# A second batch's attention placed between the first layer's units, in two PSUM banks

## The chip, the cores and the metric

The kernel runs on one core of one Trainium2 chip. The metric is the device time of one execution in microseconds; lower is better.

## The reference

Attention over two batches with 8 heads, 576 tokens and 64 values a head, then two dense layers over all 1152 tokens. Cut to what matters:

```python
q_d, k_d, v_d = means of 4 neighbouring tokens                # 144 tokens
out_up    = repeat(softmax(q_d k_d^T / 8) v_d, 4)
out_local = softmax(q k^T / 8 where |i - j| < 4) v
x = (out_up + out_local), heads side by side                  # [1152, 512]

h = x @ w_in1; P = a0 + a1 h + a2 h^2 + a3 h^3
x = (P / (1 + |b0| |h| + |b1| h^2 + 1e-6)) @ w_out1           # 512 -> 2048 -> 512
h = x @ w_in2; out = (h * tanh(softplus(h))) @ w_out2
```

## The kernel before

**Attention.** Eight steps, each of them one pair of heads of one batch (steps 0 to 3 are batch 0, steps 4 to 7 batch 1). All of it is float32. One step on TensorE (PE): `turn_q` and `turn_k` transpose q and k (L399); `score_local` makes the banded scores in 36 small products (L422); `score_down` those of the pooled tokens (L432); `turn_p` transposes the local weights (L443) and `turn_d` the pooled ones (L454); `out_down` (L463) and `out_local` (L475, 36 small products) make the outputs. ScalarE (ACT) copies each of the transposed things out of PSUM (`put`, L565) and takes the exponentials. VectorE (DVE) pools q and k (L722), adds the mask and takes off the maximum (`shift_local` L741 to L744, `shift_down` L757 and L760), sums (L766 to L768), adds the two outputs (`join`, L793) and makes the float16 rest of x (`x_rest`, L799). GpSimd (POOL) pools v and normalises (L925, L930).

**The plan.** `STAGES` names for each stage its engine and its tick within a step, a step starts every 10 ticks, and each engine's queue is this list in order of ticks. A stage that writes PSUM opens one or more jobs; the jobs take the banks 0 to 6 in turn, and a job waits until the one that held its bank before has been emptied. Bank 7 is for `keep_busy`: filler matmuls of the identity that feed nothing (L392). They stand at the start and in the first and the last step.

**Weights.** A unit is a 128 x 1024 piece of `w_in` (even numbers) or `w_out` (odd). SyncE (SP) loads it, ACT makes its float16 head (L622), DVE makes the rest of an even unit (L839), POOL that of an odd one in two halves (L938, L940). 13 units are made during the attention, the others during the first layer.

**Layers.** They begin when all eight steps are through (`x_rest_put` at 8). The tokens are cut in blocks (layer one: 256, 256, 256, 192, 192), the work in 80 tiles. For tile m, `hidden(m)` makes h in one of two banks (24 products, L498); ACT, DVE and POOL make g out of it in a chain (`first_reads`, `fraction`, `estimate`, `quotient`, `head`, `rest`); `output_first(m)` multiplies by `w_out` (L519), `output_second` in layer two (L539). PE's queue is `hidden(0..3)`, and then `output(m)`, `hidden(m + 4)` in turn. `hidden(m)` waits for `h_done` of tile m - 2, which DVE gives with the last `fraction` part (L828). At the end of a block the sums leave as the next layer's x (L676, L870).

## Time and profile before

| | us |
|---|---|
| three timed runs | 530.66, 531.88, 538.64 (median 531.88) |
| the profiled execution | 529.39, its span 527.6 |
| first matmul of the layers starts | 129.11 |
| first output of layer one starts | 147.10 |
| busy in the span: PE, DVE, ACT, POOL | 507.1, 391.0, 305.6, 194.7 |

The span goes from the first to the last instruction; the execution's time has 1.8 us more around it. PE is TensorE's matmul row, PEld its weight loads, which overlap with it. The granted clock is a share of 2.4 GHz: 1.00 is 2.4 GHz and 0.50 is 1.2 GHz. The starts of PE's rows are measured, their ends modelled, so neighbouring rows overlap a little; what a stage takes is read from start to start.

### The profile page before, as it was taken

How to read it: one execution, taken by the hardware profiler on the slowest of the kernel's cores; microseconds unless marked ns; L12 is line 12 of the kernel's file. 1: busy time of each engine (PE TensorE's matmuls, PEld its weight loads, DVE VectorE, ACT ScalarE, POOL GpSimd, SP SyncE). 2: the span in 40 equal slices, each digit the busy share in tenths (PEclk: the TensorE clock that was granted, in tenths of full speed). 3: DMA queues.
4: the chain of work that ended last, by engine and by line, in shares of the span. 5: the costliest groups of instructions: out<-in, count | busy, mean ns of one | idle time of the engine just before them, and what ended most of it. 6: DMA issues, size and time to landing. Idle time of an engine off the chain costs nothing.

```text
span 527.6 us, 11364 instructions
## 1 busy us (share of the span) xinstructions
PE 507.1 (96%) x4566; PEld 378.8 (72%) x4566; DVE 391.0 (74%) x670; ACT 305.6 (58%) x553; POOL 194.7 (37%) x204
## 2 busy tenths in 40 slices
PE   7999999999799989989999999999999999999995
PEld 5788888886588878878989989744444555557762
DVE  1687674552688887887888887887787888787873
ACT  2465463331878668786787878454545455545542
POOL 6486663320167242551542554312121222221221
PEclk8795755555899999999999999999999999999999
DMA  7999893111111211202112100000000020000101
GB/s 166 217 216 203 185 170 96 28 42 73 48 40 41 81 44 38 81 4 79 41 41 81 42 1 1 1 1 1 1 0 1 0 81 1 1 1 0 61 2 40
DMA packets 45572, 29.72 MB, mean 56 GB/s; under 512 B 30928, under 2 KB 39120, under 8 KB 45520
## 3 DMA queue, kind: packets, MB, share of 16 engines
q1 hardware_dynamic: 44344, 28.71, 22.1%
q8 instruction: 36, 0.59, 0.5%
q10 hardware_dynamic: 1176, 0.30, 0.3%
q14 instruction: 16, 0.13, 0.1%
HBM read 26.64 MB, written 2.36 MB: 55 GB/s over the span
## 4 chain that ended last, share of the span: by engine, by line
PE 50%; issue 29%; POOL 10%; DVE 5%; ACT 3%; DMA 1%; ACTq 0%; POOLq 0%; DVEq 0%
PE bank L498 15%; PE bank L519 14%; POOL g_l L953 9%; PE bank L422 5%; PE bank L475 5%; PE bank L443 3%; PE bank L399 2%; PE bank L392 2%; PE bank L432 1%; PE bank L463 1%; DMA late<-in_k 1%; PE bank L454 1%; PE bank L539 1%; ACT work L644 1%; DVE x_l L870 1%
## 5 line engine op out<-in xcount | busy, mean ns | idle before, releaser
L953 POOL TENSOR_TENSOR g_l<-work,g_h 128x512 f16<-128x512 f32 (+1 forms) x80 | 85.9, 1074 | 271.1 <-ACT g_h L668 253.4
L498 PE MATMUL bank<-x_h,w 128*128 128x256 f16 (+1 forms) x640 | 104.0, 266 | 4.6 <-DVE work L828 3.4
L519 PE MATMUL bank<-g_h,w 128*128 128x256 f16 (+1 forms) x640 | 101.2, 262 | 0.3 <-POOL g_l L953 0.3
L498 PE MATMUL bank<-x_h,late 128*128 128x512 f16 (+2 forms) x384 | 96.8, 326 | 0.0
L539 PE MATMUL bank<-late,g_h 128*128 128x512 f16 x288 | 92.1, 379 | 1.5 <-POOL g_l L953 1.5
L658 ACT ACTIVATE bank<-work,coef 128x512 f32<-128x512 f32 (+1 forms) x80 | 52.1, 652 | 69.1 <-DVE work L824 66.1
L498 PE MATMUL bank<-x_l,w 128*128 128x256 f16 (+1 forms) x320 | 85.3, 267 | 0.0
L519 PE MATMUL bank<-g_l,w 128*128 128x256 f16 (+1 forms) x320 | 83.8, 262 | 0.0
L498 PEld LDWEIGHTS bank<-x_h,w 128*128 128x128 f16 x640 | 61.9, 99 | 11.1 <-DVE work L828 4.0
L519 PEld LDWEIGHTS bank<-g_h,w 128*128 128x128 f16 x640 | 60.9, 98 | 6.6 <-issue 1.3
L498 PE MATMUL bank<-x_l,late 128*128 128x512 f16 (+2 forms) x192 | 62.6, 326 | 0.0
L814 DVE SCALAR_TENSOR_TENSOR work<-work,coef 128x512 f32<-128x512 f32 (+1 forms) x40 | 30.3, 758 | 38.7 <-ACT work L644 38.7
L565 ACT ACTIVATE late<-bank 128x288 f32<-128x288 f32 (+2 forms) x80 | 30.6, 426 | 45.4 <-PE bank L454 19.1
L498 PEld LDWEIGHTS bank<-x_h,late 128*128 128x128 f16 x384 | 37.6, 98 | 26.0
L539 PE MATMUL bank<-late,g_l 128*128 128x512 f16 x144 | 54.6, 379 | 0.0
L539 PEld LDWEIGHTS bank<-late,g_h 128*128 128x128 f16 x288 | 28.2, 98 | 34.8 <-POOL g_l L953 2.5
L848 DVE SCALAR_TENSOR_TENSOR work<-work,bank 128x512 f32<-128x512 f32 (+1 forms) x80 | 50.1, 626 | 0.0
L852 DVE SCALAR_TENSOR_TENSOR work<-work,bank 128x512 f32<-128x512 f32 (+1 forms) x80 | 49.9, 623 | 0.0
L641 ACT ACTIVATE work<-bank 128x512 f32<-128x512 f32 (+1 forms) x40 | 22.2, 555 | 45.2 <-PE bank L498 44.9
L668 ACT ACTIVATE g_h<-work 128x512 f16<-128x512 f32 (+1 forms) x80 | 47.0, 588 | 2.3 <-DVE work L861 2.2
L824 DVE SCALAR_TENSOR_TENSOR work<-work 128x512 f32<-128x512 f32 (+1 forms) x40 | 47.9, 1197 | 0.0
L817 DVE TENSOR_SCALAR work<-work 128x512 f32<-128x512 f32 (+1 forms) x40 | 16.0, 400 | 34.5 <-ACT work L649 34.5
(92 smaller groups left out, 860.0 us busy)
## 6 DMA issues: line engine op xcount, KB each, us to landing
late<-in_v SPq DMA_DIRECT2D x16, 288.0 KB
raw<-in_moe_w_out SPq DMA_DIRECT2D x8, 512.0 KB, 3.8
raw<-in_moe_w_in SPq DMA_DIRECT2D x7, 512.0 KB, 3.6
work<-in_moe_w_in SPq DMA_DIRECT2D x5, 512.0 KB, 6.4
late<-in_moe_w_out SPq DMA_DIRECT2D x5, 512.0 KB, 3.9
out<-w SPq DMA_DIRECT2D x9, 256.0 KB, 2.8
late<-in_q SPq DMA_DIRECT2D x15, 144.0 KB
late<-in_k SPq DMA_DIRECT2D x15, 144.0 KB
```

The source lines that it names most:

```text
L422: last = pe.matmul(ps[32 * g:32 * g + 32, KW * u:KW * (u + 1)], q_t[s % 2][h0:h0 + 64, QT * t:QT * (t + 1)], k_t[s % 2][h0:h0 + 64, QT * t ...
L498: last = pe.matmul(ps, w_in(l, wp)[:, kk, at], x[:, kk, t0:t0 + n], start=(kk == 0 and wp == 0 and x is x_h), stop=(kk == KD - 1 and wp == 1))
L519: last = pe.matmul(ps, w_out(0, wp)[:, f, 128 * d:128 * (d + 1)], g[q % 4][:, i * n:(i + 1) * n], start=False, stop=(f == FT - 1 and d % 2 ...
L539: last = pe.matmul(y2_bank[row % 4][:, :], g[q % 4][:, i * n + 128 * t:i * n + 128 * (t + 1)], w_out(1, wp)[:, f, :], start=(f == 0 and wp ...
L565: act.activation(dst, src, ACT.Copy, scale=scale).then_inc(act_emptied, 1)
L658: act.activation(r, den[q % 3][:, 0:w], ACT.Ln, bias=(one_eps, two)[layer]).then_inc(ln_done, 1)
L668: act.activation(g_h[q % 4][:, 0:w], num[q % 4][:, 0:w], ACT.Copy).then_inc(g_head, 1)
L814: dve.scalar_tensor_tensor(out=d, in0=d, scalar=b1_abs, in1=ab[q % 2][:, 0:w], op0=ALU.mult, op1=ALU.add).then_inc(den_done, 1)
L824: dve.scalar_tensor_tensor(out=d, in0=d, scalar=2.0, in1=d, op0=ALU.add, op1=ALU.mult).then_inc(den_done, 1)
L848: dve.scalar_tensor_tensor(out=d, in0=d, scalar=(Q_ONE, 2.0)[layer], in1=r, op0=ALU.add, op1=ALU.mult).then_inc(nt_done, 1)
L852: dve.scalar_tensor_tensor(out=d, in0=d, scalar=(2.0, 2.0 * K2)[layer], in1=r, op0=ALU.subtract, op1=ALU.mult).then_inc(nr_done, 1)
L953: pool.tensor_tensor(g_l[q % 4][:, 0:w], num[q % 4][:, 0:w], g_h[q % 4][:, 0:w], ALU.subtract).then_inc(g_rest, 1)
```

## The change

Four parts, in the code's order.

1. The plan has one list for everything: attention stages, loads, heads and rests of weight units. Each engine goes through its part of it with `Schedule.until(tick)`. The layers begin at tick 60.5 (`LAYERS`); the four units of the ramp are 0.94 ticks apart, and each slot of `output(m)`, `hidden(m + 4)` takes 2.5 ticks. Stages of later ticks stand between those units on every engine: the tails of steps 4 and 5 and nearly all of 6 and 7.
2. Jobs before tick 56.25 take banks 0 to 6 in turn, later ones banks 6 and 7 only, since the layers need 0 to 5.
3. `hidden(0)` waits for four steps of x, not eight, and tile 16, the first with tokens of batch 1, for all eight.
4. Filler matmuls follow `score_local` (3), `out_local` (3) and its first half (3) in every step that stands before the layers, and every stage of step 0 (4). In all there are 92 fillers, 84 before. `turn_p` is three jobs of 4, 4 and 1 transposes, k is loaded and turned ahead of q, and units 7 and 9 are made during the layers: five odd units in slots 1 to 5.

The diff, cut:

```diff
-    EARLY_OUT = 5
-    SLOTS = (6, 4)
+    EARLY = [0, 1, 2, 3, 4, 5, 6, 8, 10, 12, 14]
+    LATER = [7, 9, 11, 13, 15] + [FT + i for i in range(FT)]
...
+    LAYERS, PREFILL, SLOT = 60.5, 3.75, 2.5
+    TWO_BANKS = LAYERS - 4.25
...
-              ("pe", "score_down", 9),
...
+              ("pe", "score_down", 6),
...
+    def pe_tick(p):
+        return LAYERS + PREFILL + SLOT * p
+    def other_tick(m, part):
+        return max(LAYERS + PREFILL * (m + 2) / 4 + part, pe_tick(m - 3 + part))
...
-            bank = n_jobs % 7
+            if tick < TWO_BANKS:
+                bank, n_early = n_early % 7, n_early + 1
+            else:
+                bank, n_late = 6 + n_late % 2, n_late + 1
...
+            def until(self, tick):
+                while self.done < len(self.todo) and self.todo[self.done][0] < tick:
+                    _, stage, i = self.todo[self.done]
+                    stage(i)
+                    self.done += 1
...
+                    if j == 0 and PERIOD * s + 21 < TWO_BANKS:
+                        keep_busy(3)
+            def with_filler(stage, times):
+                at = next(t for _, name, t in STAGES if name == stage.__name__)
+                def run(s):
+                    stage(s)
+                    if PERIOD * s + at < TWO_BANKS:
+                        keep_busy(4 if s == 0 else times)
+                return run
...
                 if q == 0:
-                    pe.wait_ge(x_rest_put, STEPS)
+                    for bank in range(6):
+                        wait_emptied(pe, holder_at_switch[bank])
+                    pe.wait_ge(x_rest_put, PAIRS)
+                elif l == 0 and f0 == 0 and t0 + n > S:
+                    pe.wait_ge(x_rest_put, STEPS)
...
-            for _, i, s in plan:
-                if STAGES[i][0] == "pe":
-                    stages[STAGES[i][1]](s)
-                    if s == 0 or s == STEPS - 1:
-                        keep_busy(4)
+            schedule = Schedule("pe", stages)
             for m in range(LAG):
+                schedule.until(LAYERS + PREFILL * m / 4)
                 hidden(m)
             for m in range(NT):
+                schedule.until(pe_tick(m))
                 (output_first, output_second)[tiles[m][0]](m)
                 if m + LAG < NT:
+                    schedule.until(pe_tick(m + 0.5))
                     hidden(m + LAG)
```

In the changed kernel the same operations have other lines. On PE: turns L416, score_local L440, score_down L450, turn_p L459, turn_d L478, out_down L487, out_local L499, fillers L409, hidden L541, output_first L562. On DVE: pooling L771, shift_local L790 to L793, shift_down L806 and L809, join L842, x_rest L848; the fraction's parts L869, L876, L883.

PE's queue where step 2 goes over to step 3, before: the turns, the local output in two halves, turn_p.

```order
L399 MATMUL bank2<-ident,late 128x72 x4
L399 MATMUL bank3<-ident,late 128x72 x4
L475 MATMUL bank4<-late 64x32 x18
L475 MATMUL bank5<-late 64x32 x18
L443 MATMUL bank6<-ident,late 38x128 x3
L443 MATMUL bank0<-ident,late 38x128 x3
```

The same place now:

```order
L416 MATMUL bank2<-ident,late 128x72 x4
L416 MATMUL bank3<-ident,late 128x72 x4
L499 MATMUL bank4<-late 64x32 x18
L409 MATMUL bank7<-ident 128x256 x3
L499 MATMUL bank5<-late 64x32 x18
L409 MATMUL bank7<-ident 128x256 x3
L459 MATMUL bank6<-ident,late 38x128 x4
```

Fillers stand after each half of the local output.

PE's queue from turn_d(5) to the turn of k for the last step, before:

```order
L454 MATMUL bank5<-ident,late 72x72 x4
L454 MATMUL bank6<-ident,late 72x72 x4
L432 MATMUL bank0<-late 72x144
L432 MATMUL bank1<-late 72x144
...
L399 MATMUL bank2<-ident,late 128x72 x4
L399 MATMUL bank3<-ident,late 128x72 x4
```

Now, between hidden(4) and output(1):

```order
L478 MATMUL bank7<-ident,late 72x72 x4
L478 MATMUL bank6<-ident,late 72x72 x4
L450 MATMUL bank7<-late 72x144
L450 MATMUL bank6<-late 72x144
...
L416 MATMUL bank7<-ident,late 128x72 x4
L416 MATMUL bank6<-ident,late 128x72 x4
L562 MATMUL bank4<-g_h1,w1 128x256
```

Three stages that had six banks now have two, so each stage waits for the emptying of the one ahead of it.

DVE's queue at the start of the layers, before: the fraction of tile 0 behind all of the attention.

```order
L799 SCALAR_TENSOR_TENSOR x_l<-late,x_h 128x576
L889 TENSOR_SCALAR coef<-coef 128x1 x4
...
L814 SCALAR_TENSOR_TENSOR work<-work,coef 128x512
L821 TENSOR_TENSOR work<-work,bank 128x512
L828 SCALAR_TENSOR_TENSOR work<-work,coef,bank 128x512
L814 SCALAR_TENSOR_TENSOR work<-work,coef 128x512
```

Now:

```order
L869 SCALAR_TENSOR_TENSOR work<-work,coef 128x512
L842 TENSOR_TENSOR late<-bank7,late 128x288
L842 TENSOR_TENSOR late<-bank6,late 128x288
L771 TENSOR_REDUCE late<-late 128x144
L876 TENSOR_TENSOR work<-work,bank0 128x512
L883 SCALAR_TENSOR_TENSOR work<-work,coef,bank0 128x512
L869 SCALAR_TENSOR_TENSOR work<-work,coef 128x512
L897 SCALAR_TENSOR_TENSOR work<-work,bank2 128x512
L848 SCALAR_TENSOR_TENSOR x_l<-late,x_h 128x576
```

The join of step 4, the pooling of k for step 6 and x_rest(4) stand between the parts of tiles 0 and 1, ahead of the operations that give h_done.

## Rows read from the trace of the kernel before

**Rows 1.** The page: span, engine PE, and the granted clock in 40 slices

```profile
span 527.6 us, 11364 instructions
...
PE 507.1 (96%) x4566; PEld 378.8 (72%) x4566; DVE 391.0 (74%) x670; ACT 305.6 (58%) x553; POOL 194.7 (37%) x204
...
PEclk8795755555899999999999999999999999999999
```

**Rows 2.** Table of stretches: us, busy us of PE, PEld, DVE, ACT, POOL, clock, DMA share, GB/s

```profile
19.50:39.98 20.48, 19.43 (x392) 17.04 (x393) 17.36 (x36) 14.16 (x33) 17.26 (x18) 1.00 0.98 208
39.98:60.46 20.48, 20.37 (x253) 17.21 (x250) 14.10 (x29) 11.36 (x23) 15.40 (x17) 0.50 0.91 185
60.46:67.30 6.84, 6.84 (x160) 6.18 (x159) 5.04 (x12) 3.90 (x12) 1.89 (x3) 1.00 0.87 205
67.30:129.10 61.80, 60.60 (x700) 49.78 (x697) 32.18 (x71) 23.03 (x49) 20.55 (x21) 0.50 0.36 77
129.10:147.10 18.00, 14.58 (x98) 10.73 (x99) 10.43 (x21) 12.12 (x19) 3.50 (x4) 0.82 0.17 59
147.10:181.30 34.20, 34.20 (x315) 30.64 (x315) 28.13 (x40) 26.26 (x44) 17.54 (x17) 1.00 0.21 63
147.10:527.60 380.50, 369.65 (x2841) 265.36 (x2840) 306.12 (x487) 236.30 (x416) 127.93 (x121) 1.00 0.09 28
```

**Rows 3.** PE's timeline at full clock, step 2's group and what stands before it

```profile
20.79 1.16 PE L443 MATMUL bank<-ident,late 128*38 128x128 f32 x9 [0.79 <-POOL late L925]
...
28.70 2.29 PE L475 MATMUL bank<-late 38*64 38x32 f32 x72
30.92 0.61 PE L392 MATMUL bank<-ident 128*128 128x256 f16 x4
31.37 1.15 PE L443 MATMUL bank<-ident,late 128*38 128x128 f32 x9
32.44 2.39 PE L422 MATMUL bank<-late 64*32 64x38 f32 x72
34.76 0.78 PE L454 MATMUL bank<-ident,late 72*72 72x72 f32 x8
35.47 0.71 PE L432 MATMUL bank<-late 64*72 64x144 f32 x8
...
36.76 0.71 PE L463 MATMUL bank<-late 72*64 72x144 f32 x8
```

**Rows 4.** The same timeline at half clock: turn_p of two steps, one row of fillers

```profile
41.24 2.10 PE L443 MATMUL bank<-ident,late 128*38 128x128 f32 x9
...
56.99 2.11 PE L443 MATMUL bank<-ident,late 128*38 128x128 f32 x9
...
92.70 1.06 PE L392 MATMUL bank<-ident 128*128 128x256 f16 x4
93.69 1.23 PE L463 MATMUL bank<-late 72*64 72x144 f32 x8
```

**Rows 5.** Table of stretches: one attention step at full clock

```profile
24.69:34.94 10.25, 10.25 (x207) 9.02 (x208) 8.63 (x19) 6.56 (x14) 9.26 (x11) 1.00 0.93 192
```

**Rows 6.** Waits of PE: us in total, times, longest

```profile
PE bank L513 <- DVE x_l L870: 4.8, 4, 1.5
PE bank L498 <- DVE work L828: 3.4, 2, 2.4
```

**Rows 7.** Groups of instructions: DVE and ACT in the whole span, POOL in 147.1 to 181.3

```profile
L565 ACT ACTIVATE late<-bank 128x288 f32<-128x288 f32 (+2 forms) x80 | 30.6, 426 | 45.4 <-PE bank L454 19.1 <-PE bank L443 19.0 <-PE bank L399 5.4
...
L757 DVE TENSOR_REDUCE small<-bank 72x2 f32<-72x288 f32 x16 | 6.5, 446 | 2.7 <-PE bank L432 2.6
...
L839 DVE SCALAR_TENSOR_TENSOR w<-raw,w 128x1024 f16<-128x1024 f32 x3 | 3.6, 1191 | 0.0
...
L940 POOL TENSOR_TENSOR w<-raw,w 128x512 f16<-128x512 f32 x3 | 4.0, 1333 | 0.2
...
L938 POOL TENSOR_SCALAR raw<-raw 128x512 f32<-128x512 f32 x3 | 2.7, 909 | 0.0
```

More of the change, by code:

```diff
@@ L103, in attention_moe_moe @@
-    plan = sorted((PERIOD * s + t, i, s) for s in range(STEPS) for i, (_, _, t) in enumerate(STAGES))
-    JOBS = {"turn_q": 2, "turn_k": 2, "score_local": 1, "score_down": 2, "turn_p": 3, "turn_d": 2,
+    LAYERS, PREFILL, SLOT = 60.5, 3.75, 2.5
+    TWO_BANKS = LAYERS - 4.25
+    STAGES = [("sp", "load_qk", -16),
+              ("pe", "turn_k", -4),
+              ("act", "put_k", -2),
+              ("pe", "turn_q", 0),
+              ("act", "put_q", 0),
+              ("dve", "pool_q", 2),
+              ("dve", "pool_k", 3),
+              ("sp", "load_v", 4),
+              ("pe", "score_local", 4),
+              ("pe", "score_down", 6),
+              ("dve", "shift_local", 6),
+              ("act", "exp_local", 7),
+              ("dve", "shift_down", 8),
+              ("act", "exp_down", 10),
+              ("sp", "load_windows", 10),
+              ("pool", "norm_local", 10),
+              ("dve", "sum_local", 10),
+              ("dve", "sum_down", 12),
+              ("pe", "turn_p", 12),
+              ("pool", "norm_down", 14),
+              ("act", "put_p", 14),
+              ("pe", "turn_p_end", 14),
+              ("act", "put_p_end", 16),
+              ("act", "put_d", 16),
+              ("pe", "turn_d", 16),
+              ("pool", "pool_v", 17),
+              ("pe", "out_down", 19),
+              ("act", "put_down", 20),
+              ("pe", "out_local", 21),
+              ("dve", "join", 23),
+              ("act", "x_head", 23),
+              ("dve", "x_rest", 24)]
@@ L108, in attention_moe_moe @@
+    for i, u in enumerate(LATER):
+        slot = 1 + i if u < FT else 24 + 1.5 * (u - FT)
+        events += [(pe_tick(slot - 3) - 3, "sp", "load_unit", u), (pe_tick(slot - 2.25), "act", "head_unit", u),
+                   (pe_tick(slot - 2), REST_ENGINE[u % 2], "rest_unit", u)]
+    plan = sorted(events, key=lambda event: event[0])
+    JOBS = {"turn_q": 2, "turn_k": 2, "score_local": 1, "score_down": 2, "turn_p": 2, "turn_p_end": 1, "turn_d": 2,
             "out_down": 1, "out_local": 2}
-    DVE_EMPTIES = ("score_local", "score_down", "out_local")
+    EMPTIES = {"put_q": "turn_q", "put_k": "turn_k", "shift_local": "score_local", "shift_down": "score_down",
+               "put_p": "turn_p", "put_p_end": "turn_p_end", "put_d": "turn_d", "put_down": "out_down", "join": "out_local"}
@@ L119, in attention_moe_moe @@
             job = (name, s, j)
-            bank_of[job], place[job], emptied[job] = bank, n_jobs, (by, counts[by])
+            bank_of[job], place[job] = bank, n_early + n_late
             before[job] = holder.get(bank)
             holder[bank] = job
+        for j in range(JOBS[EMPTIES[name]] if name in EMPTIES else 0):
+            freed[eng] += 1
+            emptied[(EMPTIES[name], s, j)] = (eng, freed[eng])
+    holder_at_switch = {bank: job for job, bank in bank_of.items() if bank < 6}
@@ L596, in put_p, with put_p_end @@
                     act.wait_ge(job_filled, place[("out_local", s - 1, 1)])
[L597 to L599 removed]
+                put_p_job(s, "turn_p", 0, 0, 4)
+                put_p_job(s, "turn_p", 1, 4, 4)
+            def put_p_end(s):
+                put_p_job(s, "turn_p_end", 0, 8, U - 8)
             def put_d(s):
@@ L893, in _ @@
             dve.memset(ln_k, math.log(K2)).then_inc(coefs, 1)
+            schedule.until(LAYERS)
             dve.wait_ge(coefs, 8)
@@ L898, in _ @@
                 for part in range(3):
+                    schedule.until(other_tick(m, 0.6 + 0.33 * part))
                     if m < NT:
```

203 lines of the change are left out of this document (84 added, 119 removed).

## The prediction

> **What bounds the kernel now.** I read the page's first lines and its forty slices, then a table of stretches, then TensorE's and VectorE's timelines, and last the waits. [rows 1]: PE is busy for 96% of a span of 527.6 us, so nothing counts that doesn't shorten PE's own time. The clock row says how: it stands at 5 in slice 4 and in slices 6 to 10, and at 9 from slice 12 on. [rows 2] gives the same by stage. In 39.98 to 60.46 and in 67.30 to 129.10 PE is busy almost throughout (20.37 of 20.48 us, 60.60 of 61.80) at a granted clock of 0.50, the lower level (1.2 GHz); from 147.10 on it is 1.00. So up to 129.10 the attention is bound by PE at half its clock. After 147.10 the layers are bound by PE at full clock: 369.65 of 380.50 us busy.
>
> **What an attention step costs PE.** One step (two heads) at full clock, by starts in [rows 3]: nine transposes of the local weights 31.37 to 32.44 = 1.07 us; the local scores (L422) 2.32; turn_d (L454) 0.71; score_down (L432) and one turn (L399) 35.47 to 36.76 = 1.29, and out_down (L463) and the other turn, which are as long, 1.29; the local output (L475) 28.70 to 30.92 = 2.22. Sum 8.9 us. At half clock [rows 4] a step goes from 41.24 to 56.99 = 15.75 us. Eight steps are 71 us at full clock; the old kernel takes 129.1.
>
> **The change, part by part.** Three things happen: filler matmuls of ident into bank 7 stand in every step before the layers, not only in the first and last; the plan is cut at tick 60.5, where the layers begin; and what is left of the attention is put between their units, in banks 6 and 7.
>
> (1) *The stretch up to the first layer matmul.* In the old kernel turn_p (L443) of steps 0, 1 and 2 starts at 20.79, 31.37 and 41.24 [rows 3, 4]: 10.6 and 9.9 us a step at full clock, though PE needs only 8.9. VectorE explains it: in one such step (24.69 to 34.94) it is busy 8.63 of 10.25 us, and the DMA engines 0.93 of it [rows 5], 0.98 over 19.50 to 39.98 [rows 2]. In the new order turn_p(4) is followed by the rest of that group up to the second half of turn_q(6), then hidden(0). The step's price: PE 8.9 us and 9 fillers (3 after score_local, 3 and 3 around the second half of out_local; four in 31.37 - 30.92 = 0.45 us, so 0.11 each) = 9.9 us. VectorE 8.63 us with one weight rest of 1.19 (L839 [rows 7]), and two of them in steps 3 to 5, since all eight even units still go to it before the layers: about 9.8. DMA as dense as it was, since the unit loads are two a step as before; it gave 10.2 us a step. Three resources within 5% of each other queue behind each other, so I take 11.0. Bounds 10.25 (the old pace) and 12.4 (PE at half clock for a third of the time, 9.9 + 1/3 of the 7 us that half clock adds). First layer matmul: 20.8 + 4 x 11.0 + 7.1 (1.07 + 2.32 + 0.71 + 0.64 + 3 x 0.65 for out_down and two turns, 0.4 of filler; each piece from [rows 3]) = **71.9 us**, bounds 69 and 78, in place of 129.1. Gain 57.2 us.
>
> That the clock stays up there is an assumption, and the largest one. For it: from 19.50 to 39.98 it was 1.00 [rows 2] through four rows of four fillers, the last at 30.92, and it lasted 9 us beyond that one. It fell at 39.98, right after 36 small output products with a pause in them, and at 67.30, again at the end of such a row. Exactly this row is now broken by fillers. Against it: four fillers in 1 us at 92.70 [rows 4], and seven more such rows up to 127, did not lift it from 0.50.
>
> A rule speaks against the step as well. With no filler anywhere near, the clock went to 1.00 at 60.46, after 2 us of 128x128 transposes and 1.4 us of score products, and stood there for 6.84 us [rows 2]. The Trainium skill, "TensorE: Matmul & The Clock Gate", Part 4: PE-mode transpose, says the opposite of transposes: the full clock "doesn't engage" for them, as they don't count as a busy PE. By that rule the 33 transposes of a step would work against the fillers and the half clock would stay until the layers, which is rival A; the row shows that it can't hold strictly.
>
> (2) *The ramp of the layers.* Before, 129.10 to 147.10 = 18.0 us for four units, at a mean clock of 0.82 [rows 2]; four units at full clock are 4 x 2.62 = 10.5 us. The rest is waiting for h_done (3.4 us [rows 6]), the entry, and half clock. Now out_local(4) (2.22), turn_p(5) (1.07) and score_local(6) (2.32) stand in those gaps: 5.6 us of work. 10.5 + 5.6 + 0.5 = 16.6 is the floor; I keep **18.0 us**, as the third and fourth unit still wait for VectorE, which now has join(4), pool_k(6) and x_rest(4) between its fractions. Bounds 16.6 and 22. No gain in length, but 5.6 us of attention is done in it.
>
> (3) *What the layers now carry.* At PE tick 60.5 there remain 2 turns, 2 score_local, 2 score_down, 3 turn_p, 3 turn_d, 3 out_down, 4 out_local: 1.3 + 4.64 + 1.28 + 3.21 + 2.13 + 1.92 + 8.88 = 23.4 us at full clock. Less the 5.6 in the ramp: **+17.8 us**. It is spread over slots 0 to 10, about 4 slots a step. Does another engine become the bound? In 147.10 to 181.30 a tile takes 5.24 us of PE; DVE, ACT and POOL are busy 28.13, 26.26 and 17.54 of 34.20 [rows 2], that is 4.3, 4.0 and 2.7 us a tile. Four slots with a step are 21.0 + 8.9 = 29.9 us of PE, against DVE 17.2 + 7.5 = 24.7 (83%) and ACT 16.1 + 6 = 22 (74%). POOL 10.8 + 5 and, in slots 1 to 5, one odd weight unit each (2 x (0.9 + 1.33) us by L938 and L940, [rows 7]) where it had one in two: 1.2 for g's rest, 4.5 and 1.3, some 7.0 of 7.5 us. So PE stays the bound, but POOL is close to full for five slots, and some of the waits below may come from there.
>
> (4) *New waits.* The two banks cost PE a round trip wherever two stages stand together. That is so once at its worst: turn_d(5), score_down(6), turn_k(7) without a unit between them. score_down needs turn_d's banks back (two copies, 0.43 us each) and turn_k needs shift_down, four VectorE operations of 0.45 us [rows 7] behind whatever tile operation stands ahead: 1 + 3 us. turn_d(6) with score_down(7): 1 us. Behind a waiting PE stand output(1) and hidden(5), and behind these all engines. Elsewhere a unit of 2.62 us lies between, and in-order DVE, ACT and POOL will still be late at times: of the 37 late jobs I give 3 us in all. **+8 us**, bounds 2 and 20 (nearest rows: no wait over 0.8 us for a bank or a normalised tile in the old attention, and 0.98 and 2.4 us for h_done in the ramp).
>
> (5) *The rest.* 147.10 to 527.60 = 380.5 us stays, with its boundary waits (4.8 us for y, [rows 6]); the order of loads (k first, coefficients earlier) and the split 4+4+1 of turn_p move nothing that PE waits for longer than now. At nothing.
>
> Sum by the profiled execution: 71.9 + 18.0 + 17.8 + 8 + 380.5 = 496.2 us of span, and 529.39 - 527.6 = 1.8 around it: 498.0. The three timed runs lay at 530.66, 531.88 and 538.64, 1.3 us and more above the profiled one, so I forecast **499 us** as their like (-6%).
>
> **Rivals.** *A: the clock stays at half until the layers.* The fillers of 92 to 127 speak for it. A step then costs 15.75 + 9 x 0.24 = 17.9 us (a filler at half clock: 93.69 - 92.70 = 0.99 for four), PE being the bound again: 4.7 steps x (17.9 - 11.0) = +32: 531 us, no change. Partly so, one or two of five steps: 505 to 518.
> *B: the attention's jobs hold PE in the layers.* This one ends slower. Every one of the 37 jobs between PE's units needs its bank back from ACT or DVE, and its input by way of a chain DVE, ACT, DVE, POOL, each in order behind tile work; POOL's 4.5 us weight unit may stand ahead of a normalisation for which turn_p or turn_d waits. It decides from 1.4 us a job (50 us: 498 - 8 + 50 = 540, slower by 2%); at 2 us it is 564. Against it: the page of before shows 0.3 to 0.8 us for such waits on PE, and a tick is 2 to 3 us long in the layers.
> *C: better than forecast.* VectorE and the loads keep 10.25 us a step, the boundary wait after the first block is filled with steps 6 and 7, and only two of the bank waits show: 484 to 488.
>
> **How the numbers follow.** The forecast with its bounds, 488 to 505: 0.57. Partly half clock, or waits towards 20 us, 505 to 518: 0.19. A, 518 to 534: 0.10. B above 540: 0.05. C below 488: 0.09. The range 486 to 518 leaves out some 2 in 10. A measurement of this kernel tells 2%, 10.6 us, from no change; below 521 counts as faster: 0.86, same 0.09, slower 0.05.
>
> **What would show it.** The clock 1.00 in most slices from 20 us on; the first L541 at 69 to 78 us; the first L562 some 18 us after; PE busy above 96% between them and slot 11, with one wait of 3 us for shift_down (L809) at turn_k(7). A clock of 0.50 in slices 3 to 6 means A. POOL or DVE named as releaser of L459, L478, L450 or L416 in the layers, with over 1 us each, means B.

## The result, and the profile after

The changed kernel took **518.35 us** (median of four executions, 511.29 to 523.62; two more took 515.84 and 523.88) beside 531.27 us for the kernel before on the same chip: a ratio of **0.967, interval 0.960 to 0.974**. Forecast were 499 us and 486 to 518. The direction is right. The point is 19 us too low, and this median lies 0.35 us above the upper end of the range; the ratio, 0.967 of 531.27, stands for 513.7 us, which is inside it. The profiled execution took 523.14 us, at the long end of the changed kernel's times. A second profile of the same kernel, taken among the experiments, is of an execution of 514.24 us; the two are read side by side. The ratios and their intervals leave out executions more than 1.5% above the fastest of their kernel, while the medians and ranges given here are over all executions; since part of that scatter is the kernel's own clock, as will be seen, both are given.

The page of the changed kernel: span, engines, and the granted clock in 40 slices of 13.0 us.

```profile
span 521.3 us, 11406 instructions
...
PE 492.1 (94%) x4574; PEld 363.2 (70%) x4574; DVE 392.9 (75%) x670; ACT 305.6 (59%) x553; POOL 191.3 (37%) x204
...
PEclk9887655999999899999999999989999999999999
```

Beside [rows 1], PE is busy 15.0 us less and idle 8.7 us more. The clock is no longer at 5 for six slices, but it isn't at 9 from 20 us on either: it sinks from 8 in slices 2 and 3 through 7 and 6 to 5 in slices 6 and 7. Later there are two more 8s, in slices 14 and 27, which the old kernel doesn't have.

The table of stretches of the changed kernel, in the columns of [rows 2]. The cuts are 60 us, the first layer matmul (L541), the first output matmul of layer one (L562), the first output matmul of layer two (L582) and the end.

```profile
20.00:60.00 40.00, 38.91 (x620) 32.05 (x618) 29.52 (x66) 21.34 (x45) 21.97 (x25) 0.80 0.90 197
60.00:88.20 28.20, 28.20 (x318) 23.70 (x318) 15.40 (x32) 11.12 (x25) 6.64 (x8) 0.50 0.61 131
88.20:109.30 21.10, 19.42 (x255) 15.91 (x254) 14.89 (x24) 15.60 (x28) 10.12 (x11) 0.88 0.20 61
109.30:334.40 225.10, 213.42 (x2268) 187.10 (x2268) 176.37 (x289) 155.96 (x284) 90.53 (x89) 0.99 0.16 44
334.40:521.30 186.90, 178.67 (x960) 93.94 (x960) 145.98 (x235) 92.04 (x159) 49.90 (x47) 0.99 0.05 16
```

The same table of the second profile of this kernel:

```profile
20.00:60.00 40.00, 38.33 (x721) 33.00 (x723) 35.51 (x73) 25.98 (x56) 27.93 (x28) 0.96 0.90 200
60.00:82.10 22.10, 20.06 (x233) 16.57 (x230) 13.45 (x30) 8.72 (x21) 5.02 (x7) 0.59 0.85 167
82.10:101.80 19.70, 18.02 (x253) 15.15 (x251) 14.82 (x24) 15.50 (x27) 10.55 (x11) 0.94 0.23 59
101.80:325.40 223.60, 211.90 (x2267) 186.40 (x2266) 176.44 (x289) 156.09 (x284) 90.64 (x89) 1.00 0.15 45
325.40:512.40 187.00, 178.71 (x960) 94.02 (x960) 145.92 (x235) 92.16 (x160) 49.95 (x47) 0.99 0.05 16
```

And the kernel before, cut at its first output matmul of layer two (345.20), since the prediction had only the sum of the two:

```profile
147.10:345.20 198.10, 192.59 (x1881) 171.80 (x1881) 163.84 (x256) 147.39 (x260) 86.75 (x82) 1.00 0.14 41
345.20:527.60 182.40, 177.06 (x961) 93.57 (x959) 142.29 (x232) 88.91 (x157) 41.18 (x39) 1.00 0.04 14
```

So the sum of the prediction stands against the first profile like this:

| us | before | forecast | after | after, second profile |
|---|---|---|---|---|
| to the first layer matmul | 129.1 | 71.9 | 88.2 | 82.1 |
| ramp | 18.0 | 18.0 | 21.1 | 19.7 |
| layer one from there | 198.1 | 198.1 + 17.8 + 8 = 223.9 | 225.1 | 223.6 |
| layer two | 182.4 | 182.4 | 186.9 | 187.0 |
| span | 527.6 | 496.2 | 521.3 | 512.4 |

The misses are 16.3 + 3.1 + 1.2 + 4.5 = 25.1 us. Two thirds lie before the first layer matmul, in the stretch whose clock was assumed. There the fillers do break the row of output products, as meant; a piece of PE's timeline around 56 us, where the clock falls to half, shows it:

```profile
53.89 1.24 PE L499 MATMUL bank<-late 38*64 38x32 f32 x36
55.06 0.50 PE L409 MATMUL bank<-ident 128*128 128x256 f16 x3
55.49 2.03 PE L499 MATMUL bank<-late 38*64 38x32 f32 x36
57.45 0.82 PE L409 MATMUL bank<-ident 128*128 128x256 f16 x3
58.06 2.13 PE L459 MATMUL bank<-ident,late 128*38 128x128 f32 x9
```

The first 36 output products take 1.24 us, the next 36 take 2.03, and the nine transposes 2.13 instead of 1.15: the clock falls in the middle of the row, between two groups of fillers. It goes up and down: full from 21.5 to 32, 35.5 to 42 and 49 to 56 us, half between and from 56 to 93.5. The second profile has other steps (full 20 to 43.5 and 47 to 64, half until 84.5), with the same instructions in the same order.

### The profile page after: what moved, and what is told of

Its sections match the earlier page's. It is cut to its first block, busy times and chain, and to the rows that moved or that the text cites. A ratio compares the mean times of both kernels' runs of the same rounds, so it can differ in the third digit from the quotient of the medians.

```text
span 521.3 us, 11406 instructions
## 1 busy us (share of the span) xinstructions
PE 492.1 (94%) x4574; PEld 363.2 (70%) x4574; DVE 392.9 (75%) x670; ACT 305.6 (59%) x553; POOL 191.3 (37%) x204
## 4 chain that ended last, share of the span: by engine, by line
PE 50%; issue 24%; POOL 11%; DVE 7%; ACT 5%; DMA 1%; ACTq 0%; POOLq 0%; DVEq 0%
PE bank L541 17%; PE bank L562 14%; POOL g_l L1001 8%; PE bank L499 4%; PE bank L440 4%; PE bank L582 2%; PE bank L459 2%; PE bank L409 2%; PE bank L416 2%; DMA late<-in_q 1%; ACT late L673 1%; DVE x_l L919 1%; PE bank L450 1%; DVE work L869 1%; PE bank L487 1%
## 5 line engine op out<-in xcount | busy, mean ns | idle before, releaser
L562 PE MATMUL bank<-g_h,w 128*128 128x256 f16 (+1 forms) x640 | 102.6, 264 | 2.6 <-POOL g_l L1001 2.6
L541 PE MATMUL bank<-x_h,w 128*128 128x256 f16 (+1 forms) x640 | 103.5, 266 | 1.7 <-DVE work L883 1.7
L582 PE MATMUL bank<-late,g_h 128*128 128x512 f16 x288 | 92.8, 382 | 4.9 <-DVE x_l L919 2.9
L541 PE MATMUL bank<-x_h,late 128*128 128x512 f16 (+2 forms) x384 | 97.2, 327 | 0.0
L541 PE MATMUL bank<-x_l,w 128*128 128x256 f16 (+1 forms) x320 | 85.0, 266 | 0.0
L562 PE MATMUL bank<-g_l,w 128*128 128x256 f16 (+1 forms) x320 | 84.4, 264 | 0.0
L562 PEld LDWEIGHTS bank<-g_h,w 128*128 128x128 f16 x640 | 61.3, 98 | 11.8 <-POOL g_l L1001 4.4
L541 PEld LDWEIGHTS bank<-x_h,w 128*128 128x128 f16 x640 | 61.8, 99 | 7.3 <-DVE work L883 2.2
L541 PE MATMUL bank<-x_l,late 128*128 128x512 f16 (+2 forms) x192 | 62.8, 327 | 0.0
L869 DVE SCALAR_TENSOR_TENSOR work<-work,coef 128x512 f32<-128x512 f32 (+1 forms) x40 | 34.8, 870 | 32.2 <-ACT work L691 32.0
L541 PEld LDWEIGHTS bank<-x_h,late 128*128 128x128 f16 x384 | 37.7, 98 | 26.6 <-issue 0.8
L582 PEld LDWEIGHTS bank<-late,g_h 128*128 128x128 f16 x288 | 28.3, 98 | 39.1 <-POOL g_l L1001 3.6
L607 ACT ACTIVATE late<-bank 128x288 f32<-128x288 f32 (+3 forms) x80 | 31.3, 425 | 40.8 <-PE bank L478 29.0
L582 PE MATMUL bank<-late,g_l 128*128 128x512 f16 x144 | 55.1, 382 | 0.0
L879 DVE SCALAR_TENSOR_TENSOR work<-work 128x512 f32<-128x512 f32 (+1 forms) x40 | 44.7, 1117 | 0.0
L872 DVE TENSOR_SCALAR work<-work 128x512 f32<-128x512 f32 (+1 forms) x40 | 17.9, 448 | 30.8 <-ACT work L696 30.8
```

Source lines behind the costliest of these rows:

```text
L541: last = pe.matmul(ps, w_in(l, wp)[:, kk, at], x[:, kk, t0:t0 + n], start=(kk == 0 and wp == 0 and x is x_h), stop=(kk == KD - 1 and wp == 1))
L562: last = pe.matmul(ps, w_out(0, wp)[:, f, 128 * d:128 * (d + 1)], g[q % 4][:, i * n:(i + 1) * n], start=False, stop=(f == FT - 1 and d % 2 ...
L582: last = pe.matmul(y2_bank[row % 4][:, :], g[q % 4][:, i * n + 128 * t:i * n + 128 * (t + 1)], w_out(1, wp)[:, f, :], start=(f == 0 and wp ...
L607: act.activation(dst, src, ACT.Copy, scale=scale).then_inc(act_emptied, 1)
L869: dve.scalar_tensor_tensor(out=d, in0=d, scalar=b1_abs, in1=ab[q % 2][:, 0:w], op0=ALU.mult, op1=ALU.add).then_inc(den_done, 1)
L879: dve.scalar_tensor_tensor(out=d, in0=d, scalar=2.0, in1=d, op0=ALU.add, op1=ALU.mult).then_inc(den_done, 1)
```

## The experiments

All ratios are against the kernel before in the same set of runs, whose medians were 530.15, 530.47 and 532.5 us. In the first of these sets (no_fill, fill8, units_early, old_fill) the old kernel itself scattered: six of its 17 executions took 517.95 to 524.98 us, at a mean granted clock of 0.922 to 0.941 over the span, and the others 528.04 to 540.19 us at 0.886 to 0.916. The ratios of that set lean on the shorter ones (fill8's is 0.973, where the medians give 0.967), so they are not compared to the per cent with ratios of the other two sets. The milestones of a run (first layer matmul, ramp, layer one, layer two) are those of the table above, from its profile.

**Do the fillers hold the clock, or does nothing?** The first run leaves out the added fillers (those of step 0 stay, as in the old kernel); the second puts eight where three stood.

```
no_fill                                          fill8
- keep_busy(3)                                   - keep_busy(3)
+ keep_busy(3 if s == 0 else 0)                  + keep_busy(8)
- score_local=with_filler(score_local, 3)        - score_local=with_filler(score_local, 3)
+ score_local=with_filler(score_local, 0)        + score_local=with_filler(score_local, 8)
- out_local=with_filler(out_local, 3)            - out_local=with_filler(out_local, 3)
+ out_local=with_filler(out_local, 0)            + out_local=with_filler(out_local, 8)
```

> The changed kernel without its fillers from step 1 on (step 0 keeps its fours). Theory 1, the clock: the profiled execution lost 16 us to my forecast ahead of the layers because PE ran at 0.50 from 56 to 93 us in spite of the fillers. If the fillers buy any clock at all, taking them away puts the half clock over nearly all of 31 to 93 us: first layer matmul at 92 to 100 us, time 520 to 530. Rival 1, the fillers buy nothing and only cost PE time (9 a step, 0.24 us each at half clock): first layer matmul 4 to 8 us earlier than 88 us, time 505 to 515.

Measured: 519.4 us, ratio 0.985 (0.976 to 0.995); first layer matmul at 85.3. Without fillers the first layer matmul comes 2.9 us earlier than in the first profile with them and 3.2 us later than in the second. It lies between the two forecasts (92 to 100 us, and 4 to 8 us before 88). The stretches of this kernel:

```profile
24.00:41.00 17.00, 17.00 (x347) 14.85 (x344) 14.15 (x31) 10.99 (x25) 13.64 (x15) 0.99 0.81 196
41.00:85.30 44.30, 44.30 (x531) 37.88 (x530) 28.96 (x66) 20.45 (x44) 13.49 (x15) 0.50 0.79 163
```

and its PE timeline at the end of its longest stretch at full clock:

```profile
32.15 0.61 PE L409 MATMUL bank<-ident 128*128 128x256 f16 x4
32.60 1.15 PE L459 MATMUL bank<-ident,late 128*38 128x128 f32 x9
33.67 2.38 PE L440 MATMUL bank<-late 64*32 64x38 f32 x72
...
39.27 2.96 PE L499 MATMUL bank<-late 38*64 38x32 f32 x72
```

Four groups of step 0 stand between 25.9 and 32.8; from there on there is no filler, and for 8 us more only transposes and small products run, at a mean of 0.98; only the last part of the 72 output products at 39.27 slows down (2.96 us where full clock gives 2.29, [rows 3]). So this small work can keep the clock for a while by itself. From 20 us to its first layer matmul this execution was at half clock for 48 us, more than in six of the seven profiles with nine fillers a step (14 to 44 us, table further down); by the line through those, 48 us would put the first layer matmul at 90 us. So the 33 fillers that are left out here seem to have bought some clock and to have cost about as much PE time, 4 to 8 us at 0.11 to 0.24 us each.

> The changed kernel with 8 fillers in place of 3 at each of the three places of a step. Theory 1: a denser PE keeps 1.00 for most of the stretch; PE then needs 8.9 + 24 x 0.11 = 11.6 us a step and the first layer matmul stands at 74 to 80 us, time 505 to 512 with little scatter. Rival 1, the filler does not hold the clock: a step at half clock is 15.75 + 24 x 0.24 = 21.5 us, first layer matmul beyond 98 us, time 525 to 540.

Measured: 512.64 us, ratio 0.973 (0.964 to 0.982); 508.45 profiled. Its stretches:

```profile
20.00:74.70 54.70, 54.65 (x1000) 47.34 (x999) 43.90 (x96) 31.78 (x70) 29.49 (x31) 1.00 0.93 205
74.70:93.30 18.60, 16.92 (x253) 14.58 (x253) 15.12 (x26) 15.67 (x28) 11.11 (x11) 1.00 0.32 82
93.30:319.70 226.40, 214.94 (x2268) 187.98 (x2268) 176.30 (x289) 155.94 (x284) 90.70 (x89) 0.98 0.15 43
319.70:506.60 186.90, 178.68 (x960) 93.98 (x960) 145.93 (x235) 92.06 (x159) 49.88 (x47) 0.99 0.04 16
```

This is the assumption of step (1) made true: the clock is 1.00 from 20.5 us through the ramp. The steps take 11.7 us (turn_p at 31.85, 43.55, 55.22, 66.92) with 24 fillers, where I had put 11.0 with nine; the first layer matmul comes at 74.7. The ramp, 21.1 us at 0.88, is 18.6 at 1.00. Layers one and two are as in the changed kernel, so what they lose has nothing to do with the clock of the attention. But three of its six times are above 515 us (515.27, 517.47, 523.19). The mean granted clock over the span is on record for each execution: 0.969, 0.962 and 0.959 for these three, 0.978 to 0.985 for the other three. So it is the clock that varies, and even eight fillers hold it in some executions only.

**More groups of fillers instead of thicker ones.** A group of three or four behind every PE stage, 30 a step.

```
- keep_busy(4 if s == 0 else times)
+ keep_busy(4 if s == 0 else 3)
```

> The changed kernel with 3 fillers behind every stage of every step before the layers (30 a step, not 9). Theory 1b: the fillers hold the clock if none of the small products goes on for long without them; then the clock is 1.00 from 20 us on, a step costs 8.9 + 3.3 = 12.2 us and the first layer matmul stands at 76 to 82 us in every execution: times 507 to 514, a scatter of some 5 us. If the clock still falls, a step at half clock is 23 us and times go up to 540.

Measured: 515.2 us, ratio 0.967 (0.962 to 0.973); first layer matmul 81.4. The theory fails: the clock still fell twice (at 44.5 and at 58 us, for 3.5 us each), and one execution took 569.28 us at a mean granted clock of 0.836. A step at full clock is about 12.6 us long (turn_p at 32.51 and 45.07), where 12.2 were expected. 24 fillers in thick groups did better in the profile (74.7); against nine (77.1 to 93.2 in seven profiles) thirty show no clear gain or loss.

**The other half of the change: fillers without interleaving.** The old kernel, whose attention is finished before the layers, with fillers in steps 1 to 6: three, and eight. (As the code cut shows, the group within out_local stands in all eight steps.)

```
 for j in range(2):                 # out_local of the old kernel
+    if j == 0:
+        keep_busy(3)               # 8 in the other run
...
+ elif STAGES[i][1] in ("score_local", "out_local"):
+     keep_busy(3)                  # 8 in the other run
```

> The old kernel with only the fillers of the change (3 after score_local, 3 within and 3 after out_local in steps 1 to 6). Theory 1, with mixed clock as in the changed kernel (1.00 for some 60% of 20 to 60 us and then half): attention ends 5 to 15 us earlier, time 517 to 527. If the fillers do nothing for the clock: 6 x 9 x 0.24 = 13 us longer, 540 to 545. From this and the changed kernel follows what the interleaving alone is worth.

Measured: 524.35 us, ratio 0.966 (0.955 to 0.977), but single executions from 505.73 to 539.26; the medians over all executions give 0.989. Its shortest execution is below the shortest of the interleaved kernel with the same nine fillers (507.17 of twelve), and its median above both of that kernel's (518.35, 514.27). The profiled one (537.65) had the first layer matmul at 138.0, later than without fillers, as a part of its stretches shows:

```profile
21.00:79.00 58.00, 58.00 (x642) 47.55 (x642) 28.45 (x59) 23.49 (x49) 31.90 (x35) 0.50 0.74 164
79.00:86.00 7.00, 7.00 (x144) 5.94 (x140) 4.96 (x12) 4.15 (x11) 0.71 (x2) 0.98 0.40 113
86.00:138.00 52.00, 49.62 (x760) 41.07 (x760) 31.49 (x71) 22.03 (x49) 20.72 (x21) 0.76 0.30 69
```

58 us at 0.50 with the same nine fillers a step that I had counted on. An execution of 505.73 us of the same program is 32 us shorter; it left no trace, but its mean granted clock was 0.976, where the profiled one had 0.911. Nine fillers don't hold the clock reliably.

> The old kernel, attention whole ahead of the layers, with 8 fillers at the three places of steps 1 to 6. It tells what the interleaving is worth once the clock holds: 20.8 + 7 x 11.6 + 10 = 112 us to the first layer matmul, 18.0 of ramp and 380.5: 510 to 515. The changed kernel with 8 fillers had a median of 512.6. So I expect the two to be within 1%: the interleaving gains some 37 us ahead of the layers and gives back 29 in layer one and 4.5 in layer two.

Measured: 516.46 us, ratio 0.971 (0.966 to 0.977); 513.35 profiled.

```profile
20.00:114.50 94.50, 92.74 (x1640) 79.23 (x1638) 65.23 (x141) 47.91 (x107) 54.24 (x56) 0.96 0.70 150
114.50:131.00 16.50, 13.09 (x98) 10.02 (x98) 10.41 (x21) 12.11 (x19) 3.47 (x4) 0.90 0.20 65
131.00:329.20 198.20, 192.66 (x1882) 171.80 (x1882) 163.92 (x256) 147.60 (x260) 86.75 (x82) 1.00 0.14 41
329.20:511.50 182.30, 177.01 (x961) 93.58 (x959) 142.27 (x232) 88.91 (x157) 41.23 (x39) 1.00 0.04 14
```

Against fill8 this gives what interleaving is worth where fillers hold the clock in both: the first layer matmul comes 39.8 us earlier, and it is paid back with 2.1 us in the ramp, 28.2 in layer one and 4.6 in layer two. 4.9 us of span are left, and 3.8 us between the medians (512.64 and 516.46, from two sets of runs), 0.7%; the two ratios, 0.973 and 0.971, don't tell them apart. These 4.9 us are not idle time that was filled: PE is idle for 26.8 us of fill8's span and for 20.5 of this one, 6.3 more. It is busy for 479.8 us in place of 491.0, and 92 fillers fewer (152, not 244; 0.11 us each) are 10.1 of these 11.2 us. The work moved runs on PE either way; with the clock held, interleaving saves only fillers.

**Where layer one and two lose.** Here I had several candidates: layer-two units prepared too late or in the wrong place (three runs), the five odd units of layer one that crowd POOL and ACT in slots 1 to 5, and turn_k(7) directly behind score_down(6).

```
- slot = 1 + i if u < FT else 24 + 1.5 * (u - FT)
+ slot = 1 + i if u < FT else 16 + 1.4 * (u - FT)          # units_early
+ slot = 1 + 1.5 * i if u < FT else 24 + 1.5 * (u - FT)    # odd_spread
+ slot = 1 + i if u < FT else 14 + 2 * (u - FT)            # units_two
+ slot = 1 + i if u < FT else 15 + 2 * (u - FT)            # units_odd
```

> The changed kernel, but layer two's 16 weight units are made in slots 16 to 37 of the plan, not 24 to 46.5. In the profiled execution PE stood still for 2.5 us in 290 to 300 and 3.4 us in 329 to 345, with a unit's head on ACT in the chain both times; the old kernel had finished its units by then. Theory 2: the late units cost layer one's end and layer two's start 4 to 6 us; time 506 to 512. Rival 2: the same stalls come with the units wherever they stand (the old kernel had 10.9 us of them over the layers), time unchanged within 2 us.

Measured: 527.78 us, ratio 0.999 (0.990 to 1.008). The windows of its layers:

```profile
99.20:334.60 235.40, 217.38 (x2267) 189.99 (x2267) 182.73 (x293) 159.40 (x286) 99.41 (x97) 0.97 0.15 44
334.60:517.00 182.40, 177.04 (x961) 93.59 (x959) 142.34 (x232) 88.88 (x157) 41.21 (x39) 1.00 0.04 14
```

Layer two is back at the 182.4 of the old kernel, to the tenth: the 4.5 us that it loses in the change are those of units prepared in slots 24 to 46, some of which run into it. By the two tables 2.9 of them are PE idle (8.2 us, 5.3 in the old kernel) and 1.6 PE busy for longer: behind the wait of 2.95 us at 338.77 the granted clock is 0.76 over 340 to 345. But layer one is 10.3 us longer than in the change, a larger price than the one saved: 6.3 us of it idle, with waits for g_l of up to 3.7 us, and 4.0 busy at a mean clock of 0.97. Both forecasts fail, since the stalls moved with the units and grew.

> The changed kernel with units 7, 9, 11, 13 and 15 at slots 1, 2.5, 4, 5.5 and 7 in place of 1 to 5. In the first profile output(2) started at 124.84, after a chain put_d on ACT, weight head, two weight halves and pool_v on POOL (115.6 to 123.6), then g's rest; PE stood for 2.3 us in 109.3 to 125. Theory 3 (POOL's queue): the wait goes for the most part, from first output of layer one to first of layer two 221 to 223 us in place of 225.1. Rival 3 (the wait comes from PE's own stall at the two banks, which started the chain late): 224 to 226 us.

Measured: 519.99 us, ratio 0.971 (0.967 to 0.974); layer one 227.3 us, layer two 186.9. Spreading the odd units saves nothing in layer one (2.2 us more than in the change). The theory that they crowd it falls. The trace of the changed kernel had said so: in 115.6 to 124.8, where POOL works through the two halves of such a unit and a pooling, PE waited for POOL only 0.22 us.

The waiting rows of PE's timeline in layer one of the changed kernel are few (the group in brackets is the idle time before the row):

```profile
115.88 0.71 PE L450 MATMUL bank<-late 64*72 64x144 f32 x8 [0.67 <-ACT late L607]
...
117.99 0.74 PE L416 MATMUL bank<-ident,late 72*128 72x72 f32 x8 [1.40 <-DVE late L809]
...
124.84 0.28 PE L562 MATMUL bank<-g_h,w 128*128 128x256 f16 x1 [0.22 <-POOL g_l L1001]
...
148.13 0.71 PE L450 MATMUL bank<-late 64*72 64x144 f32 x8 [0.67 <-ACT late L607]
...
171.30 1.11 PE L556 MATMUL bank<-zeros 32*128 32x512 f16 x2 [2.58 <-DVE x_l L919]
```

The 1.40 us is the wait that step (4) named, turn_k(7) for the subtractions of shift_down, at half its forecast price. The next run puts turn_k(7) 1.5 ticks and put_k(7) one tick later.

```
+ shift = {("turn_k", 7): 1.5, ("put_k", 7): 1}
- events = [(PERIOD * s + t, eng, name, s) ...
+ events = [(PERIOD * s + t + shift.get((name, s), 0), eng, name, s) ...
```

> The changed kernel with turn_k of the last step 1.5 ticks later, behind output(1) and no longer directly behind score_down(6), and put_k a tick later. Theory 4: of my 5 us for the two-bank round trips only 2.7 us were seen (0.67, 1.40, 0.67); moving the turn takes away the 1.40 and at most what hangs on it: the stretch from first output of layer one to first of layer two 222 to 224 us. Rival 4: POOL's chain is the later of the two, nothing changes (225 us).

Measured: 521.44 us, ratio 0.966 (0.962 to 0.971); layer one 226.9 us. The wait itself is gone, and others have come, further down the same timeline:

```profile
117.82 0.67 PE L417 MATMUL bank<-ident,late 72*128 72x72 f32 x8
...
122.44 0.71 PE L488 MATMUL bank<-late 72*64 72x144 f32 x8 [1.32 <-issue]
...
123.51 0.28 PE L563 MATMUL bank<-g_h,w 128*128 128x256 f16 x1 [0.36 <-POOL g_l L1002]
```

1.40 us removed; 1.32 us are new, and the wait for g_l has grown from 0.22 to 0.36. The wait was a place where PE waited for the slower engines, not the cause of their being late.

**Preparation of layer-two units behind the copies of a block end.** The chain of work at the start of layer two in the changed kernel (start, us, what) shows why PE waits there:

```profile
333.51 0.44 ACT x_h L723
...
334.25 1.07 ACT late L673
...
335.49 1.00 issue
...
337.78 0.95 DVE x_l L919 x2
...
338.77 2.59 PE bank L582 x6
```

L723 is the copy of the block's new x on ACT; directly behind it in ACT's queue stands L673, the rounded head of a weight unit, 1.07 us. The harm is done on VectorE, in the time that this chain calls issue. Its queue has the rest of that unit (L855) ahead of the last work on the tile and of the block's x_l (L919):

```profile
335.35 1.23 DVE L855 SCALAR_TENSOR_TENSOR late<-raw,late 128x1024 f16<-128x1024 f32 x1 [2.59 <-ACT late L673]
```

DVE stands for 2.59 us until the head is there, works 1.23 us on the rest, and only then goes on to what PE needs. PE's L582 waits 2.95 us in the end. If this is a mechanism, then units in slots 14, 16, ... 44, which put such a head behind the copies at four of five block ends, should lose in layer one, and units in slots 15, 17, ... 45, with none there, should not.

> The changed kernel with layer two's units at every second slot, 14 to 44, not every 1.5 slots from 24. With units at 16 + 1.4 k layer two took 182.4 us as in the old kernel, but layer one 235.4 in place of 225.1. Theory 5, density: ACT needs 3.3 us a tile of 192 tokens and 1.05 us a unit against 3.97 us of PE, so a unit every 1.5 tiles makes ACT and DVE the bound there and one in two tiles does not: layer one 220 to 224 us, layer two 182 to 185, together 4 to 8 us less than 412. Rival 5, place: units in the slots that follow the attention hurt whatever their spacing, and layer one is 228 us or more.

Measured: 532.2 us, ratio 0.989 (0.983 to 0.994); layer one 240.4, layer two 185.7. PE's waits in this kernel (total, times, longest):

```profile
PE bank L556 <- DVE x_l L919: 12.0, 4, 3.5
PE bank L562 <- POOL g_l L1001: 5.0, 6, 1.5
```

> The changed kernel with layer two's units at every second slot as before, but at 15, 17, ... 45, so that no weight head comes directly behind the ACT copies that end a block (it did at four of five block ends of layer one with 14, 16, ... 44). Theory 6, collision: a unit's head (1.05 us on ACT) behind the end of a block delays the next tile's h_done, the y rest and g's rest, and that, not the density, made layer one 240.4 us; now layer one 218 to 222 us, layer two 182 to 184, so the time from first layer matmul to the end is 422 to 427 us against 430 to 433 in the changed kernel. Theory 5 (density alone): the same 240 us, as the density is the same.

Measured: 515.59 us, ratio 0.966 (0.960 to 0.972); layer one 229.4, layer two 183.2.

```profile
PE bank L556 <- DVE x_l L919: 6.5, 4, 2.6
...
PE bank L562 <- POOL g_l L1001: 2.0, 2, 1.0
```

One slot's shift of the same work takes 11.0 us off layer one. The two waits fall by 8.5 us (12.0 to 6.5 and 5.0 to 2.0); PE's whole idle time in it falls by 6.5 (19.9 to 13.4), and its busy time by 4.5 (220.5 to 216.0), at mean clocks of 0.96 and 0.98. Density alone would have changed nothing, so the collision is real and costs about 2 us a block end (8.5 over four) and what follows of lower clock. As in the changed kernel it is VectorE's queue that passes it on. At the second block end units_two has the unit's rest between the tile's work and x_l, and in units_odd no unit stands there:

```profile
215.89 1.23 DVE L855 SCALAR_TENSOR_TENSOR late<-late 128x1024 f16<-128x1024 f32 x1 [1.77 <-ACT late L673]
...
218.36 1.28 DVE L919 SCALAR_TENSOR_TENSOR x_l<-bank,x_h 128x512 f16<-128x512 f32 x2
```

The runs don't separate the head on ACT from the rest on DVE, since a shift moves both. But I had expected 218 to 222 us of layer one, and 229.4 came; so theory 6 names a cause and overrates it. Layers one and two together are 412.6 us here and 412.0 and 410.6 in the two profiles of the changed kernel: the change as it was has a head behind the copies at one block end only, so there was little to save. The late places cost 4.5 us in layer two, the earlier ones 4.3 in layer one.

**The best of both, and the changed kernel once more.** units_odd with the eight fillers of fill8:

> The same with 8 fillers in place of 3 at the three places of a step. With the first layer matmul at 75 to 85 us, as with 8 fillers before, and 422 to 427 us behind it: 500 to 512 us. If theory 6 fails it is 508 to 523 as with 8 fillers alone.

Measured: 509.38 us (504.81 to 515.57), ratio **0.956 (0.951 to 0.962)**; first layer matmul 77.3, ramp 18.6, layers 229.3 and 183.1. It has the lowest median of all kernels run. Its parts explain it: the start of fill8, the layers of units_odd. In the same set of runs old_fill8, with everything before the layers, has 0.971 (0.966 to 0.977), so interleaving together with the moved units is worth 1.5% by the ratios and 3.2 us by the profiles' spans.

> The changed kernel as it is, beside its variants on one chip. Theory 1: the place of the half clock ahead of the layers differs from execution to execution, so the first layer matmul stands anywhere from 72 to 92 us, the rest of the span (from there to the end) stays within 2 us of the 433 us of its first profile; times 508 to 525, median 518.

Measured: 514.27 us, ratio 0.962 (0.957 to 0.968), with the second profile shown above. It is 4 us below the first median of the same kernel. The first layer matmul at 82.1 is within the forecast; the rest of the span, 430.3 us, is 2.8 us from the 433.1 of the first profile, a little more than the 2 expected.

## Why the prediction was right, and what of it was not

**What bounds the kernel** was read correctly: PE is busy in 94% of the span, and whatever changed the time changed PE's time: its clock, or its waits at the block ends.

**Step (1), the stretch to the first layer matmul: the assumption that the clock stays up failed; the price did not.** It named the assumption as its largest, and rival A in part (505 to 518, a chance of 0.19) is what happened, at its far end. The measured time is near the end of the range for that reason: the range was wide enough for the miss, the sum was not right. The runs allow a test of both prices. Take the kernels with nine fillers a step and plot the first layer matmul against the time at half clock between 20 us and that matmul, read from the granted clock of each trace:

| | odd_spread | units_early | after, second | after | turnk_moved | units_two | units_odd |
|---|---|---|---|---|---|---|---|
| half clock, us | 13.6 | 17 | 21.6 | 44.2 | 41.9 | 37 | 57.2 |
| first layer matmul, us | 77.1 | 79.0 | 82.1 | 88.2 | 88.4 | 85.7 | 93.2 |

All seven have the same instructions up to there, but for the place of a few weight units. A straight line through them rises by 0.35 us per us of half clock and meets 73.2 us at none. I had 71.9, and 17.9 us a step at half against 11.4 at full clock gives (17.9 - 11.4)/17.9 = 0.36. The 17.9 is measured twice, at half clock throughout: turn_p at 40.22 and 58.11 in old_fill, at 38.44 and 56.32 in units_odd. The 11.4 is a step of the second profile (turn_p at 32.42 and 43.82; I had taken 11.0), and it has a wait of 1.10 us for v's transfer in it; PE alone would need about 10.1 us, an estimate from fill8's 11.7 less 15 fillers of 0.11. So the working of the step stands, and the 16.3 us are 44.2 us of half clock at 0.35 (15.5) and the 1.3 by which the line's foot lies above 71.9, less 0.5 by which this profile lies under the line.

I gave the fillers more weight than the rows did. The eight rows of four that did not lift the clock between 92 and 127 us [rows 4] were stronger evidence than the stretch before 39.98, where it had not yet fallen; no_fill shows that this stretch needed no filler for its last 8 us.

The rule of the Trainium skill ("TensorE: Matmul & The Clock Gate", Part 4: PE-mode transpose), that the full clock doesn't engage for transposes, would have given the right sign of the miss, but the trace doesn't agree with it: in no_fill the clock stayed at 0.98 for 8 us of transposes and small fp32 products behind the last filler, and 24 to 41 us ran at 0.99.

**Step (2), the ramp**: 21.1 and 19.7 us for 18.0. With the clock held it is 18.6 (fill8, odd_fill8, fill_spread). The miss is again mostly half clock, which lasts until 93.5 us, 5 us into the ramp. That half clock could run into it wasn't in the step.

**Steps (3) and (4), attention and waits in layer one: 25.8 us forecast, 27.0 measured; right in size, half wrong in place.** PE's busy time rises by 213.42 - 192.59 = 20.8 us, of which 17.8 are the attention; 1.8 are 20 us at a clock of 0.91 after the first block end (160 to 180); 1.2 us I can't assign. PE's idle time rises by 6.2 us, not 8: the waits between two neighbouring stages in two banks are 0.67 + 1.40 + 0.67 = 2.7 where I had 5, and 3.5 come at the block ends and behind them (the first L556 waits 2.58 us where the old kernel's waited 1.51; three waits of L562 for g_l, 2.4 us, where the old kernel has one of 0.3), where VectorE and ACT are late with the end of a block. **Rival B falls**: some 30 late jobs in layer one (36 by my own list in step (3), not 37, less 6 in the ramp) with 2.7 us of bank waits are 0.1 us a job, not 1.4.

**Step (5), "at nothing": wrong by 4.5 us.** The split of turn_p shows no wait of its own. The order of loads is not free where PE is fast: in the second profile PE stands 1.10 us (until 40.54) and 2.04 us (until 64.30) before L499 for v's transfer, in odd_spread 1.98 us. The plan now asks for that transfer 11 ticks ahead of out_local, where it was 17; the old order shows no such wait, not even in old_fill8 at a clock of 0.96. No run moves the load alone. The place of layer two's units has the largest price: layer two is 186.9 in place of 182.4, and exactly 182.4 with the units earlier. What I missed is that a moved unit brings instructions of its own into the in-order queues of ACT and of DVE or POOL, and that near a block end the rest on DVE waits for the head on ACT and stands before the x_l that PE waits for.

The direction would have come out the same with the mechanism read as it is now, but for a smaller reason. The change holds two things. Where fillers hold the clock in both kernels, interleaving saves 4.9 and (with the units moved) 3.2 us by the profiles' spans, and the fillers that it spares (10.1 us) are more than that. The rest comes from the clock of the attention, as far as the profiles show: there is less of it before the layers that can run at half clock (at half clock all the way from 20 us the line above puts the first layer matmul at 73.2 + 0.35 (t - 20) = t, so at 102 us, where the old kernel's came at 129 and, in old_fill, at 138).

**Still open.** What exactly keeps or drops the clock in these streams of small products isn't settled: nine fillers a step, none, and 30 in thin groups gave overlapping paths, and 24 in thick groups held it in the profile while three of six executions were still above 515 us. Pauses of PE are a rival that no run tests alone: in the second profile the clock fell 3 us behind the pause of 1.10 us and right at the end of the one of 2.04, and in odd_spread and units_early 2 us behind pauses of 1.98 and 1.79; from 20.5 us to the first layer matmul fill8 has neither a pause of 0.2 us or more nor a fall. But other falls have no such pause ahead (67.3 us in the old kernel, 56 in the first profile, both in fill_spread). The mean granted clocks show that executions of one program differ by their clock; why, they can't tell, since only the profiled one of each leaves a trace.

## What to carry to other kernels

Where a stage runs at a clock that isn't certain, price it at both levels and give the time at each level as a term of its own; fillers count only once several executions have shown that they hold the clock. Moving small work of the bounding engine between its large work takes none of that engine's time away; here it saved only slow clock and fillers, and PE's idle time rose by 6 us, where other engines are late and at the ends of blocks. Before moving a preparation step "for free", list what stands behind each of its instructions in each in-order queue, above all next to the copies that end a block.

## What the runs showed of the hardware that was not expected

- TensorE kept the full clock for 17 us (0.99 over 24 to 41 us in no_fill), the last 8 of them without any dense half-precision matmul, only fp32 transposes and small products (64x38, 64x144, 72x144, 38x32). The 6.84 us at full clock in the old kernel [rows 2] are of the same kind.
- The granted clock took another path in two executions of one and the same program: half for 21.6 and for 44.2 us before the first layer matmul. With fillers in groups of three in the old kernel six executions lay between 505.7 and 539.3 us, 6.6% apart, at mean clocks of 0.976 and 0.890.
- One execution of no_fill took 1621.76 us among others between 515 and 532; its mean granted clock is given as 1.00, so it isn't the clock; nothing in a trace explains it, and the median hardly feels it.
